# The last chunk's routing logits taken from g through a product w_out · w_gate made on chip, with the second half of its back products handed out inside the first search

## The reference, cut to what matters

```python
# 1. linear attention: state[t+1] = w * state[t] + k v, y = r (state + u k v); 4 batches, 8 heads, 768 tokens, 48 dims
x = attention(r, k, v, w, u)                       # (3072, 384)
# 2. feed-forward, 384 -> 2048 -> 384
h = x @ w_in
g = np.maximum(h, 0.0) + alpha * np.minimum(h, 0.0)
x2 = g @ w_out
# 3. mixture of 8 experts, each takes cap = 3072 / 8 = 384 tokens
logits = x2 @ w_gate                               # (3072, 8)
order = np.argsort(-logits.flatten())              # the best pairs (token, expert) first
#    a pair is taken when its token is free and its expert not yet full
out[mask_e] = np.maximum(x2[mask_e] @ w1[e], 0.0) @ w2[e]
```

## Time and profile before

| what | value |
|---|---|
| median of 3 executions | 808.72 us (808.45 to 809.99) |
| span of the profiled execution | 808.1 us |
| PE busy | 770.3 us, 95% |
| DVE busy | 500.5 us, 62% |
| POOL busy | 474.9 us, 59% |
| ACT busy | 220.1 us, 27% |

### The profile page before, as it was taken

One profiled execution on the slowest core, in us unless ns is written; L12 is line 12 of the kernel. 1 busy time (PEld: TensorE's weight loads), 2 busy tenths in 40 slices (PEclk: granted clock), 3 DMA queues, 4 the chain that ended last, 5 costly groups with the idle time before them and its releaser, 6 DMA issues.

```text
span 808.1 us, 15970 instructions
## 1 busy us (share of the span) xinstructions
PE 770.3 (95%) x6320; PEld 649.6 (80%) x6320; DVE 500.5 (62%) x1038; ACT 220.1 (27%) x452; POOL 474.9 (59%) x471
## 2 busy tenths in 40 slices
PE   6899999999999999999999999939999999999997
PEld 4578888888888888888888888726887988989996
DVE  8877766556655565556655334477787777776221
ACT  1233322111211121112111211204244344353451
POOL 6899985555555555555554333107477775775871
PEclk8999999999999999999999999958999999999999
DMA  7865522222221222222000000014523605517401
GB/s 213 228 197 155 150 70 70 69 69 70 67 67 63 66 67 63 64 64 67 11 11 11 11 11 10 14 54 168 186 74 144 215 20 198 171 45 272 159 11 49
DMA packets 46569, 75.17 MB, mean 93 GB/s; under 512 B 6256, under 2 KB 31856, under 8 KB 46496
## 3 DMA queue, kind: packets, MB, share of 16 engines
q1 hardware_dynamic: 37776, 56.07, 22.1%
q10 hardware_dynamic: 5584, 8.46, 3.7%
q0 software_dynamic: 3136, 9.64, 3.4%
HBM read 64.71 MB, written 9.44 MB: 92 GB/s over the span
## 4 chain that ended last, share of the span: by engine, by line
PE 81%; DVE 11%; POOL 2%; issue 2%; ACT 2%; DMA 1%; SPq 0%; POOLq 0%; DVEq 0%; ACTq 0%
PE bank L1312 23%; PE bank L1314 22%; PE bank L1313 21%; PE bank L1329 3%; PE bank L1363 3%; PE bank L1346 2%; DVE grid L1205 2%; PE bank L1422 2%; PE bank L1505 2%; DVE grid L1203 1%; POOL gl L493 1%; PE bank L1564 1%; DVE both L860 1%; PE bank L1382 1%; DVE xel L1120 1%
## 5 line engine op out<-in xcount | busy, mean ns | idle before, releaser
L493 POOL TENSOR_TENSOR gl<-g,gh 128x512 fp32r<-128x512 f32 x96 | 128.2, 1336 | 202.4 <-ACT gh L667 202.2
L1003 DVE TENSOR_SCALAR q<-bank,alpha_sb 128x512 f32<-128x512 f32 x96 | 71.9, 749 | 146.2 <-PE bank L1314 146.0
L667 ACT CAST gh<-g 128x512 fp32r<-128x512 f32 x96 | 59.6, 621 | 335.4 <-PE bank L1314 298.8
L1312 PE MATMUL bank<-gh,wout_h 128*128 128x512 f32 x288 | 118.7, 412 | 1.2 <-DVE vs L887 0.4
L1312 PE MATMUL bank<-xTh,win_h 128*128 128x512 f32 x288 | 113.1, 393 | 0.3 <-DVE xTl L896 0.3
L1314 PE MATMUL bank<-gh,wout_l 128*128 128x512 f32 x288 | 112.8, 392 | 0.0
L1313 PE MATMUL bank<-gl,wout_h 128*128 128x512 f32 x288 | 112.4, 390 | 0.0
L1314 PE MATMUL bank<-xTh,win_l 128*128 128x512 f32 x288 | 112.2, 389 | 0.0
L1313 PE MATMUL bank<-xTl,win_h 128*128 128x512 f32 x288 | 112.0, 389 | 0.0
L599 POOL TENSOR_TENSOR w1l<-raw,w1h 128x384 fp32r<-128x384 f32 x64 | 65.1, 1016 | 38.4 <-ACT w2h L731 37.9
L1312 PE MATMUL bank<-xeh,w1h 128*128 128x384 f32 x192 | 69.6, 362 | 0.0
(11 more groups left out here) (203 smaller groups left out, 1453.6 us busy)
## 6 DMA issues: line engine op xcount, KB each, us to landing
raw<-w SPq DMA_DIRECT2D x32, 768.0 KB
rt<-rT SPq DMA_DIRECT2D x48, 96.0 KB, 2.9
vs<-v SPq DMA_DIRECT2D x48, 96.0 KB, 3.0
vn<-v SPq DMA_DIRECT2D x24, 192.0 KB, 2.9
x2rows<-x2n SPq DMA_DIRECT2D x23, 192.0 KB, 1.9
kt<-kT SPq DMA_DIRECT2D x44, 96.0 KB, 2.5
...
```

The costliest lines, as they stand in the source:

```text
L493: nc.gpsimd.tensor_tensor(gl[:, f % 2], g[:, f % 2], gh[:, f % 2].bitcast(F32), ALU.subtract).then_inc(gl_ready, 1)
L667: nc.scalar.copy(gh[:, f % 2], g[:, f % 2]).then_inc(gh_ready, 1)
L1003: nc.vector.tensor_scalar(q[:, f % 2], h, 0.0, alpha_sb[:, f:f + 1], ALU.min, ALU.mult).then_inc(q_ready, 1)
L1312: nc.tensor.matmul(o, a_h, b_h, start=first, stop=False)
```

## The change

**Logits from g.** (g w_out) w_gate is computed for the last chunk as g (w_out w_gate). `w_outT`, w_out transposed by the host, is loaded by SP late in chunk 4 in three transfers of 1 MB (`woT`). In the last chunk PE forms the product by `gate_product(k)`, k = 0 to 2, each four fp32 matmuls of 32 weight columns by 512 columns, which write the four partition quarters of bank 6. ACT copies it out (`wcT`), PE turns it (`turn_gate`), DVE copies it (`wc`). `score(n)` is again four such matmuls, and adds four blocks of g into the quarters of bank 5: `score(0)`, `(1)`, `(2)` inside the chunk, `score(3)` after the last g. ACT copies the sum (`lgT`), and four matmuls by `pick` add the quarters and turn the logits to token rows. DVE holds the last 8 blocks of g (`RING`).

**Back products by token rows.** In the last chunk `back_rows(f)` has the tokens as weights and `w_out` as moving operand: 12 matmuls of 128 x 384 in place of 9 of 128 x 512, and the result is token rows, without `x2T` and transposes. Blocks 0 to 8 run inside the chunk. Blocks 9 to 15 (`KEPT` = 9), 84 matmuls, are issued by `kept_back(n)`: 10 before the first counts, 3 before the logit matmuls, 12 behind them, and then inside the rounds of the first search.

**Around it.** The four `output_tile` of chunk 4 stand at f = 1 to 4 (before at 1, 5, 9, 13); `homes` at f = 5 (before 12) and the ranking of the 20 known token tiles at f = 7 and 8 (before 14 and 15); the `busy` matmuls between last chunk and search are gone; the first search counts in bank 3; SP's loading of expert weights waits for the last `hidden`; buffers lie elsewhere in SBUF.

```diff
+KEPT = 9
+RING = 8
...
+        def g_of(c, f):
+            if c < LAST or f % RING < 2:
+                return g[:, f % 2]
+            return g_more[:, f % RING - 2]
+        def gh_of(c, f):
+            return kept_h[:, f - KEPT] if c == LAST and KEPT <= f < NF - 2 else gh[:, f % 2]
+        def gl_of(c, f):
+            return kept_l[:, f - KEPT] if c == LAST and KEPT <= f < NF - 2 else gl[:, f % 2]
+        def rows_bank(b):
+            return banks[(7, 0, 1, 2)[b]]
+        def count_bank(p):
+            return banks[3 if p == 0 else 5]
...
+                if b == B - 1:
+                    sp.wait_ge(diagv_ready, NT)
+                    sp.wait_ge(kpad_ready, NT)
+                    sp.wait_ge(s_updated, 8 * LAST + 4)
+                    for k in range(KD):
+                        sp.dma_start(woT[:, k], w_outT[k * P:(k + 1) * P]).then_inc(woT_loaded, 16)
...
-            sp.wait_ge(x2n_done, NT)
+            sp.wait_ge(h_done, NF * NCH)
...
+                if c == LAST:
+                    act.wait_ge(kept_done, b + 1)
+                    rows = rows_bank(b)[:, 0:DM].rearrange("p (k t) -> p k t", k=KD)
                 else:
+                    act.wait_ge(x2n_done, B * c + b + 1)
...
+            def last_chunk():
+                for f in range(NF):
+                    act.wait_ge(g_ready, NF * LAST + f + 1)
+                    act.wait_ge(out_done, NF * LAST + min(f - 1, KEPT))
+                    if f == KEPT:
+                        act.wait_ge(gate_done, KD)
+                    nc.scalar.copy(gh_of(LAST, f), g_of(LAST, f)).then_inc(gh_ready, 1)
+                    if 1 <= f <= B:
+                        out_rows(LAST - 1, f - 1)
+                    if f == 3:
+                        act.wait_ge(gate_done, KD)
+                        nc.scalar.copy(wcT[:], banks[6][:, 0:TB]).then_inc(wcT_ready, 1)
+                act.wait_ge(scored, NF // B)
+                for half in range(2):
+                    cols = slice(half * TB // 2, (half + 1) * TB // 2)
+                    nc.scalar.copy(lgT[:, cols], banks[5][:, cols]).then_inc(lgT_ready, 1)
+                for b in range(B):
+                    out_rows(LAST, b)
...
+                if i < LAST or f < 2:
+                    wait(dve, gl_ready, NF * i + f - 1)
+                elif f == 2:
+                    dve.wait_ge(s_updated, 8 * NCH)
+                elif f >= RING:
+                    dve.wait_ge(gl_ready, NF * i + f - RING + 1)
+                    dve.wait_ge(scored, (f - RING) // B + 1)
+                nc.vector.scalar_tensor_tensor(out=g_of(i, f), in0=h, scalar=0.0, in1=q[:, f % 2], op0=ALU.max, op1=ALU.add).then_inc(g_ready, 1)
+            def last_chunk():
                 for f in range(NF):
...
+                    relu_alpha(LAST, f)
+                    if 1 <= f <= B:
+                        out_logits(LAST - 1, f - 1)
+                    if f == 4:
+                        dve.wait_ge(wc_turned, 1)
+                        nc.vector.tensor_copy(wc[:].rearrange("p m c -> p (m c)"), banks[6][:, 0:TB]).then_inc(wc_ready, 1)
+                    if f == 5:
+                        nc.vector.tensor_reduce(pick[:], ident.rearrange("p (t r) -> p r t", t=B)[:, HALF // 2 - E:HALF // 2], AX_X, ALU.add).then_inc(wc_ready, 1)
+                        homes()
+                    if f == 7:
+                        known_best()
+                    if f == 8:
+                        known_grid()
...
+            nc.vector.tensor_copy(logits[:, KNOWN:NT].rearrange("p b e -> p (b e)"), banks[4][:, 0:B * E]).then_inc(logits_ready, B)
...
+            def gate_product(k):
+                pe.wait_ge(woT_loaded, 16 * KD)
+                if k == 0:
+                    pe.wait_ge(s_summed, B * LAST)
+                for t in range(B):
+                    mm = nc.tensor.matmul(banks[6][t * HALF // 2:(t + 1) * HALF // 2, 0:TB], id_wg[:, k, P + E - HALF // 2:P + E], woT[:, k, t * TB:(t + 1) * TB],
+                                          start=(k == 0), stop=(k == KD - 1))
+                mm.then_inc(gate_done, 1)
+            def turn_gate():
+                pe.wait_ge(wcT_ready, 1)
+                for m in range(B):
+                    mm = nc.tensor.transpose(banks[6][:, m * P:(m + 1) * P], wcT[:, m * P:(m + 1) * P], ident)
+                mm.then_inc(wc_turned, 1)
+            def score(n):
+                if n == 0:
+                    pe.wait_ge(wc_ready, 1)
+                    pe.wait_ge(logits_ready, KNOWN + OUT_PRE)
+                    pe.wait_ge(x2n_ready, KNOWN + OUT_PRE)
+                pe.wait_ge(g_ready, NF * LAST + B * n + B)
+                for m in range(B):
+                    mm = nc.tensor.matmul(banks[5][m * HALF // 2:(m + 1) * HALF // 2, 0:TB], wc[:, m, n * HALF // 2:(n + 1) * HALF // 2], g_of(LAST, B * n + m),
+                                          start=(n == 0), stop=(n == NF // B - 1))
+                mm.then_inc(scored, 1)
+            def back_rows(f):
+                if f == 0:
+                    pe.wait_ge(x2t_act, 2 * LAST)
+                    pe.wait_ge(x2t_dve, LAST)
+                pe.wait_ge(gl_ready, NF * LAST + f + 1)
+                for b in range(B):
+                    rows = slice(b * P, (b + 1) * P)
+                    mm = product3(rows_bank(b)[:, 0:DM], gh_of(LAST, f)[:, rows], gl_of(LAST, f)[:, rows], wout_h[:, f], wout_l[:, f], f == 0, False)
+                mm.then_inc(out_done, 1)
+            def kept_back(n):
+                for _ in range(n):
+                    b, at = divmod(kept_at[0], 3 * (NF - KEPT))
+                    kept_at[0] += 1
+                    if b == B:
+                        return
+                    f, which = KEPT + at // 3, at % 3
+                    if b == 0:
+                        pe.wait_ge(gl_ready, NF * LAST + f + 1)
+                    rows = slice(b * P, (b + 1) * P)
+                    mm = nc.tensor.matmul(rows_bank(b)[:, 0:DM], (gl_of if which == 2 else gh_of)(LAST, f)[:, rows], (wout_l if which == 1 else wout_h)[:, f],
+                                          start=False, stop=(at == 3 * (NF - KEPT) - 1))
+                    if at == 3 * (NF - KEPT) - 1:
+                        mm.then_inc(kept_done, 1)
+            def last_chunk():
+                for f in range(NF):
+                    hidden(LAST, f)
+                    if 1 <= f <= B:
+                        output_tile(LAST - 1, f - 1)
+                    if 1 <= f <= KD:
+                        gate_product(f - 1)
+                    if f == 4:
+                        turn_gate()
+                    if 2 <= f < KEPT + 2:
+                        back_rows(f - 2)
+                    if f == 6:
+                        score(0)
+                    if f == 8:
+                        score(1)
+                    if f == 12:
+                        score(2)
...
+                        if i > 0:
+                            kept_back(2)
...
+            kept_back(10)
             pe.wait_ge(search_consts, NSEARCH)
-            pe.wait_ge(g_ready, NF * NCH)
+            pe.wait_ge(g_ready, NF * NCH - 1)
             pe.wait_ge(early_ready, 2)
-            pe.wait_ge(logits_ready, KNOWN + OUT_PRE)
             for i in range(KNOWN // 2):
-                count_pair(i)
-            busy(2, banks[3])
-            pe.wait_ge(x2t_act, 2 * c + 2)
-            pe.wait_ge(x2t_dve, c + 1)
-            pe.wait_ge(logits_ready, B * c + OUT_PRE)
+                count_pair(0, i)
+            score(NF // B - 1)
+            kept_back(3)
             for b in range(B):
-                for k in range(KD):
-                    mm = nc.tensor.matmul(banks[7][:, b * E:(b + 1) * E], x2T[:, k, b * P:(b + 1) * P], wg[:, k],
-                                          start=(b == 0 and k == 0), stop=(b == B - 1 and k == KD - 1), skip_group_check=True)
-                if b == 1:
-                    busy(1, banks[3])
+                pe.wait_ge(lgT_ready, 1 + b // 2)
+                mm = nc.tensor.matmul(banks[4][:, b * E:(b + 1) * E], lgT[:, b * P:(b + 1) * P], pick[:], start=(b == 0), stop=(b == B - 1), skip_group_check=True)
             mm.then_inc(logits_done, 1)
-            def last_rows(b):
-                if b >= 2:
-                    pe.wait_ge(x2n_ready, B * c + b - 1 + OUT_PRE)
-                for k in range(KD):
-                    mm = nc.tensor.transpose(banks[3 + b % 2][:, k * P:(k + 1) * P], x2T[:, k, b * P:(b + 1) * P], ident)
-                mm.then_inc(x2n_done, 1)
-            last_rows(0)
-            last_rows(1)
...
+                kept_back(2)
                 digit(0, m)
-                if m in (1, 2):
-                    last_rows(m + 1)
+                kept_back(6 if m < 2 * V3 else 3 * B * NF)
```

186 lines of the change are left out of this document (98 added, 88 removed).

## The result

The changed kernel takes 811.13 us (median of 8 executions, 810.58 to 811.86), the kernel before 808.69 us on the same chip (808.08 to 809.99): a ratio of 1.0026, interval 1.0017 to 1.0035. The change made the kernel slower by 2.4 us, and the forecast of 803.1 us was wrong in its sign.

What follows compares the result with a forecast made beforehand. PE, busy for 95% of the span, was taken as the bound. Step 1 adds 0.2 us, Step 2 takes off 5.8, Step 3 and Step 4 cost 0: 5.6 us shorter, span 802.5, time 803.1 us, range 799 to 810.

Steps and rivals of the forecast that it cites:

- Step 1: Last chunk up to H, the end of its last `hidden` matmul: 0.2 us later, PE not waiting inside.
- (A): Rival on the fp32 groups: one cycle per column, 3.9 us more gained, 799.3 us; chance 0.12.
- (B): Rival on the fp32 groups: array quarters run one after another, 810 to 820.6 us; chance 0.06 near 810, 0.11 above.
- Step 2: From the last `hidden` matmul's end to the logits' copy: 4.95 us in place of 10.75, a gain of 5.8 us.
- Step 3: Rounds of the first search: kept matmuls hidden at 2.4 GHz, cost 0.
- Rival (C): Kept matmuls hold up the search rounds at 1.2 GHz, losing 6 us: 809.1 us; chance 0.06 with other round delays.
- Step 4: After the last digit: last rows' store lands 2.8 us after issue, 0 to 0.3 us show, cost 0.
- Rival (D): Last rows come late, numbering and inversion move by up to 1.5 us: 804.6 us; chance 0.60 together with the forecast.

Runs made afterwards that it cites:

- weights_after_rows: Changed kernel, but SP asks for the first expert's weights only when the last rows' store has landed: 810.7 us, ratio to before 1.0016.
- old_places: Changed kernel with every operand of the chunks' products back at its place of before, expert buffers left moved: 808.89 us, ratio to before 0.9996.
- layout_only: Kernel before with only the changed kernel's order of buffers in SBUF, the experts' included: 813.0 us, ratio to before 1.005.
- early_old: Changed kernel with all 84 kept matmuls issued ahead of the last digit and the chunks' operands at their old places: 802.98 us, ratio to before 0.9941.
- low_x_moved: Kernel before with nine small buffers placed between xTh and xTl, so xTl, x2T, x2n and q lie 11,840 bytes higher: ratio to before 1.0061.
- x_up_192: Kernel before with 192 bytes left free ahead of xTh, so xTh, xTl, x2T, x2n and q lie higher: ratio to before 1.0080.

## Why the prediction was wrong

**Step 1 was right.** The last chunk takes 62.49 us, 0.29 more than before (0.2 forecast), and PE doesn't wait in it. The term of which no row existed, the group of four fp32 products into four quarters of the array, was forecast at 1.2 us. The first such group in the last chunk (timeline of PE):

```profile
456.54 1.07 PE L1524 MATMUL bank<-woT,id_wg 128*32 128x512 f32 x8
457.53 0.50 PE L1404 MATMUL bank<-xTh,win_h 128*128 128x512 f32 x1
457.87 0.39 PE L1405 MATMUL bank<-xTl,win_h 128*128 128x512 f32 x1
```

Eight records of 512 columns lie in 0.99 us, start to start. One after another each would have had 0.124 us, less than the 0.227 of an fp32r product with as many columns; so the quarters worked side by side. The product behind it takes 0.34 us to the next start, 0.11 more than its pitch. What entering costs shows at the group at 506.64:

```profile
506.33 0.39 PE L1406 MATMUL bank<-xTh,win_l 128*128 128x512 f32 x1
506.64 0.62 PE L1543 MATMUL bank<-g,wc 128*32 128x512 f32 x2
```

The product ahead of it takes 0.31 to 0.32 us to the group's start, 0.09 more than its pitch. That makes 1.2 us a group, as forecast, and rivals (A) and (B) fall by it. The estimate worked out from the Trainium skill's page TensorE: Matmul & The Clock Gate, "Measured speedup vs the span model", was 1.3 us; the row is nearer to my 1.2.

**Step 2 was right.** From H to the logits' copy it is 4.65 us (514.10 to 518.75), 4.95 forecast:

```profile
517.16 0.65 ACT L743 COPY lgT<-bank 128x256 f32<-128x256 f32 x2 [0.89 <-PE bank L1543]
...
517.66 0.99 PE L1699 MATMUL bank<-pick,lgT 128*128 128x8 f32 x8
...
518.75 0.19 DVE L1199 COPY logits<-bank 128x32 f32<-128x32 f32 x1 [3.13 <-PE bank L1699]
```

**Step 3 was right**: 13.16 us from first to last digit, at a clock of 1.00. Rival (C) didn't come about, since its clock of 1.2 GHz didn't.

**Step 4 failed**, at "it lands 2.8 us later". I took the landing from a store that had no such loads beside it, and asked of the moved store only who waits for it, not what else is under way when it moves. The weight loads follow the last digit D by about 3 us, and the kept matmuls behind the digit put the store at D + 2.9, right ahead of them. The store then took 6.6 us, and of the 5.1 us lost between the last digit and the inversion 3.8 are its landing (6.6 - 2.8).

The other 1.3 us remain where the store lands in 2.8 us: `weights_after_rows` has the inversion at D + 6.46, before had D + 5.13. Step 4 had 0.3 us of that and missed 0.9 between the end of ACT's copy and the store's issue. ACT's last copy in the changed kernel, and the one before the change:

```profile
536.50 0.48 ACT L702 COPY x2n<-bank 128x384 f32<-128x384 f32 x1 [4.88 <-PE bank L1569]
```

```profile
529.85 0.48 ACT L650 COPY x2n<-bank 128x384 f32<-128x384 f32 x1 [2.14 <-PE bank L1543]
```

It ends at D + 2.0, as forecast, but POOL issues the store at D + 2.9 (537.87). Before, it was the same 0.9 us, from 530.33 to 531.22. Rival (D) had priced up to 1.5 us, but by luck: its reason, a landing counted from the end of the 1.2 us of issuing, doesn't hold, since in `weights_after_rows` the numbering starts 3.0 us behind the issue's start.

Of DMA: Bandwidth & Descriptors, "Anatomy of one DMA", the Trainium skill says that the wait for the receipt of a write can be surprisingly long, above all when it goes to HBM. It names no load beside the write. Here the loads decide: 6.5 and 6.6 us just ahead of two of them, in four kernels, and 2.8 in every other kernel, where these came 1.6 us later or more. No run shows which part of the store's way they lengthen.

**A term was missing from the sum**: the buffers' places. The change said that buffers lie elsewhere, and I costed that at nothing without a sentence on it. The moves ahead of the chunks' operands cost 2.0 us in chunks two to five, and 2.2 to 2.4 us in the whole of the changed kernel (`old_places`). The Trainium skill's page SBUF — State Buffer, "SBUF: two separate sides", says that on the engines' side only the port pair shared by two of them causes waiting, and that PE never waits on anyone. By that rule a place would cost nothing, and the pitches of 227.1 and 232.7 ns by the same instructions speak against taking it as a rule for pace; they do not show what PE waits for.

Together: gained 6.1 us from H to the first digit and 0.3 in the search and behind the inversion, lost 5.1 behind the last digit, 2.0 in the chunks, 0.3 in the last chunk and 0.7 in the experts' stretch (246.7 us from first expert matmul to the last of PE before, 247.4 after). That sums to 1.7 us slower; the ratio says 2.1 and the medians 2.4.

The experts' 0.7 us are in part the places too. The mean time from start to start of the 128 x 384 expert products is 175.5 to 175.6 ns in all nine kernels whose expert buffers were moved, `layout_only` among them, and 174.5 to 174.7 in all eight where they stayed. But `early_old`, with 175.5, has a stretch of 246.6 us and `old_places`, with 175.6 and the same buffers, one of 247.4; what shortens the former isn't known. These products also limit the finding of the table: before, `w1h` started at 192 in a block of 256 bytes and the operand xeh that it meets at 0; after, both start at 0, and xeh by `w1h` went from 172.8 to 174.9 ns. One offset wasn't the better place here.

**What stays open** is why a start 64 bytes off in 256 slows the chunks' products. The weights for the next matmul are loaded while one runs, and both are read from SBUF; that these two reads meet is an idea that no run tested, and the slow products of unmoved operands in `low_x_moved` and `x_up_192` speak against it as the whole story. Nor was a distance smaller than 64 bytes tried.
